# The beginning of an attention and MLP kernel, laid out anew: smaller loads, another order on every engine, more bank pairs, identity matmuls at the start

## Chip, core and metric

One core of a Trainium2 chip runs the program. The metric is the device time of one execution in microseconds (us), as the median of several. "Span" is the time from the first to the last instruction of one profiled execution.

## What is computed

Three stages, all float32. B = 8 batches, 8 heads, 576 tokens, head size 64; 4608 tokens of width 512.

```python
def sm_attn(qq, kk, vv): ...      # softmax(qq kk^T / 8) vv, per batch and head
p_packed = sm_attn(p, k, v)       # 32 packed queries
x = sm_attn(q, p_packed, p_packed)
xn = x / sqrt(mean(x * x) + 1e-6) * rms_g
g = xn @ w_gate                   # 512 x 1536
x = (g * sigmoid(g) * (xn @ w_val)) @ w_o       # 1536 x 512
out = (((x @ w1) * (x @ w2)) @ w3) @ w_out      # 1024 wide inside
```

## The kernel before, in words

Each float32 operand of a large product is split into two parts of a type that TensorE takes in one pass: `hi` is a cast by ScalarE (ACT), `lo` is the difference to the original, by VectorE (DVE). A product is then three matmuls: hi·hi, hi·lo, lo·hi.

**The main loop** (L639 to L648) goes over 8 batches, 2 halves of 288 tokens and 12 chunks of the inner width. A slot is `into` (12 matmuls: gate and value of a chunk, psum banks 0 and 1), then `outof` of the slot before (12 matmuls, banks 2 to 5) and at most one **item**, a small piece of the attention of this or the next batch. ACT and DVE make the activation between them. After the loop come the two 1024-wide products (`into2`, `outof2`).

**Items** run in a written order (`FIRST_ITEMS` and `SLOT_ITEM`), and all use the same pair of psum banks, 6 and 7. `xy_full` counts items that TensorE (PE) has finished, `xy_free` those that have been read out. S1 is the scores of the packed queries, AT their transposes, PV the product with v, PT another transpose, S2 the second scores, Z and SS the sums of squares, M (six for each batch) the product of the packed values with a piece of w_gate or w_val. M pieces are split into `m_hi` (ACT) and `m_lo` (DVE), which is what `into` multiplies with.

**The inverse rms** goes from engine to engine: SS on PE, `ssum` and `ms` on DVE (L831, L836), two small operations on GpSimd (POOL, L414 and L418) that give `rr`, a store of `rr` to memory and a load spread over 128 partitions as `r_sb` (`spread_r`, L278 and L282, both issued by SyncE, SP), the scaling of `a2T` on POOL (L425), then `a2_hi` on ACT (L696) and `a2_lo` on DVE (L894). `into` of the first slot waits for `a2_lo` (L534).

**The beginning** (L611 to L638) is what is changed. w3 · w_out is multiplied out once to a 1024 x 512 matrix, in two halves of 4 banks each; `fuse(half, c)` is one step of 12 matmuls of 512 columns, and there are 8 steps for each half. Between the steps stand the items of batch 0 and the first two of batch 1. `fuse_split` (ACT L701, L703; DVE L900, L903) makes hi and lo of chunk c of w_out (`wout`, half 0 only) and of w3 (`w3a`, `w3b`). `wf_evict` reads a finished half out of psum, `store_wf` writes it to memory. `wo_split` splits chunk f of w_o, which is loaded into the region of the fuse operands once `fuse_done` says that both halves are through (L323).

All DMAs are issued by SP in one written order (L301 to L330) and go through one queue. In the beginning that is: k and p of batch 0, w_out and w3 in loads of two chunks (512 KB), v, q, then k and p of batch 1, w3's second half, four pieces of w_gate and w_val (`w_in`, 1 MB each, four buffers), v and q of batch 1, the first store of the product, `spread_r(0)`, two more w_in pieces, and w_o in three loads of 1 MB.

## Time and profile before

| what | value |
|---|---|
| median of 3 runs | 1412.66 us (1412.58 to 1413.02) |
| the profiled execution, whole | 1412.07 us |
| its span | 1410.3 us |
| mean granted TensorE clock | 0.999 of full |
| TensorE busy | 1386.3 us, 98% of the span |
| DVE, ACT, POOL busy | 43%, 29%, 10% |
| moved by DMA | 129.13 MB, 92 GB/s on average |

The rows further down come from one profiled execution. Times are from the start of the span. A row of the timeline gives the start, the duration, engine, source line, operation, what it writes and reads, and in square brackets the idle time of that engine ahead of it and what ended this idle time. Matmuls are pipelined, so a listed duration is longer than the distance to the next start; the distance is what counts. Most float32 matmuls outside the split products appear as two instructions each.

### The profile page before, as it was taken

Reading aid. Unit: us, or ns where it says so; the run is one execution under the profiler, and the core shown is the slowest. Engines: PE = TensorE matmul, PEld = TensorE weight load, DVE = VectorE, ACT = ScalarE, POOL = GpSimd, SP = SyncE. Lnnn points to the kernel's source line nnn. Section 1 sums busy time; section 2 is a strip of 40 time slices with the busy share of each in tenths; the row PEclk is TensorE's granted clock in tenths of the full one; section 3 lists DMA queues with packets and bytes.
Section 4 is the critical chain, followed back from the end, with each engine's and each line's share of the span. In section 5 each row is a group of like instructions: output and inputs, shape, how many; then the busy total and the mean of one; then the engine's idle time right before and its main releaser. Section 6 shows DMA issues by size and latency. Waiting matters only on the chain.

```text
span 1410.3 us, 22634 instructions
## 1 busy us (share of the span) xinstructions
PE 1386.3 (98%) x9688; PEld 1194.8 (85%) x9688; DVE 605.7 (43%) x1095; ACT 406.9 (29%) x803; POOL 141.4 (10%) x137
## 2 busy tenths in 40 slices
PE   7989999999999999999999999999999999999999
PEld 5679899898898998988989988888888888888887
DVE  3657556565565565655655632212212111212111
ACT  4253342433423424334233422111111111111111
POOL 0100100001001000010012030220202020202000
PEclk9999999999999999999999999999999999999999
DMA  9882451533424515323024130101011010100000
GB/s 332 233 314 82 129 163 41 196 106 93 165 86 128 163 39 197 107 92 131 18 69 167 47 107 0 60 0 60 0 60 45 16 60 0 60 0 30 0 30 30
DMA packets 59155, 129.13 MB, mean 92 GB/s; under 512 B 3504, under 2 KB 12720, under 8 KB 57264
## 3 DMA queue, kind: packets, MB, share of 16 engines
q1 hardware_dynamic: 59056, 127.70, 27.6%
q8 instruction: 76, 1.25, 0.4%
q14 instruction: 23, 0.19, 0.0%
HBM read 106.69 MB, written 20.99 MB: 91 GB/s over the span
## 4 chain that ended last, share of the span: by engine, by line
PE 95%; DVE 3%; ACT 1%; issue 1%; DMA 0%; SPq 0%; DVEq 0%; ACTq 0%
PE psum L586 9%; PE psum L584 9%; PE psum L585 9%; PE psum L546 8%; PE psum L565 7%; PE psum L567 7%; PE psum L566 7%; PE psum L547 7%; PE psum L548 7%; PE psum L606 5%; PE psum L605 5%; PE psum L604 5%; PE psum L513 3%; PE psum L500 1%; PE psum L526 1%; PE psum L467 1%
## 5 line engine op out<-in xcount | busy, mean ns | idle before, releaser
L546 PE MATMUL psum<-a_hi,m_hi 128*128 128x288 f32 x768 | 240.7, 313 | 0.4
L565 PE MATMUL psum<-g_hh,wo_hi 128*128 128x288 f32 x768 | 227.4, 296 | 4.5 <-DVE g_res L921 2.6
L547 PE MATMUL psum<-a_lo,m_hi 128*128 128x288 f32 x768 | 226.7, 295 | 0.0
L548 PE MATMUL psum<-a_hi,m_lo 128*128 128x288 f32 x768 | 226.3, 295 | 0.0
L567 PE MATMUL psum<-g_hh,wo_lo 128*128 128x288 f32 x768 | 226.0, 294 | 0.0
L566 PE MATMUL psum<-g_hl,wo_hi 128*128 128x288 f32 x768 | 225.9, 294 | 0.0
L1012 DVE TENSOR_TENSOR b_h<-b_s,psum 128x512 f32<-128x512 f32 x72 | 49.5, 688 | 408.9 <-PE psum L586 408.9
L584 PE MATMUL psum<-xh,w_hi 128*128 128x512 f32 x576 | 224.1, 389 | 0.0
L585 PE MATMUL psum<-xl,w_hi 128*128 128x512 f32 x576 | 224.1, 389 | 0.0
L586 PE MATMUL psum<-xh,w_lo 128*128 128x512 f32 x576 | 224.1, 389 | 0.0
L546 PEld LDWEIGHTS psum<-a_hi,m_hi 128*128 128x128 f32 x768 | 144.4, 188 | 50.6 <-issue 46.6
L565 PEld LDWEIGHTS psum<-g_hh,wo_hi 128*128 128x128 f32 x768 | 144.1, 188 | 7.6 <-issue 6.1
L787 ACT CAST g_hh<-g_h 128x288 fp32r<-128x288 f32 x192 | 83.2, 433 | 223.2 <-DVE g_h L982 223.2
L547 PEld LDWEIGHTS psum<-a_lo,m_hi 128*128 128x128 f32 x768 | 144.9, 189 | 0.7
L548 PEld LDWEIGHTS psum<-a_hi,m_lo 128*128 128x128 f32 x768 | 144.7, 188 | 0.0
L567 PEld LDWEIGHTS psum<-g_hh,wo_lo 128*128 128x128 f32 x768 | 144.2, 188 | 0.0
L566 PEld LDWEIGHTS psum<-g_hl,wo_hi 128*128 128x128 f32 x768 | 144.1, 188 | 0.0
L976 DVE SCALAR_TENSOR_TENSOR g_s<-g_s,psum 128x288 f32<-128x288 f32 x192 | 86.4, 450 | 124.4 <-ACT g_s L783 122.7
L586 PEld LDWEIGHTS psum<-xh,w_lo 128*128 128x128 f32 x576 | 108.1, 188 | 22.4
L585 PEld LDWEIGHTS psum<-xl,w_hi 128*128 128x128 f32 x576 | 108.1, 188 | 22.4
L584 PEld LDWEIGHTS psum<-xh,w_hi 128*128 128x128 f32 x576 | 108.1, 188 | 22.3
L796 ACT COPY b_s<-psum 128x512 f32<-128x512 f32 x72 | 42.4, 589 | 275.2 <-PE psum L586 275.2
(109 smaller groups left out, 1737.2 us busy)
## 6 DMA issues: line engine op xcount, KB each, us to landing
w_in<-in_w_gate SPq DMA_DIRECT2D x24, 1024.0 KB, 5.3
w_in<-in_w_val SPq DMA_DIRECT2D x24, 1024.0 KB, 5.3
kT<-in_kT SPq DMA_DIRECT2D x8, 1152.0 KB, 7.7
v_sb<-in_v SPq DMA_DIRECT2D x8, 1152.0 KB, 7.2
qT<-in_qT SPq DMA_DIRECT2D x16, 576.0 KB, 3.8
y_scratch<-g_res SPq DMA_DIRECT2D x16, 576.0 KB, 3.2
x_raw<-y_scratch SPq DMA_DIRECT2D x9, 1024.0 KB, 7.6
out<-b_res SPq DMA_DIRECT2D x8, 1024.0 KB, 5.2
```

The source lines that it names most:

```text
L546: nc.tensor.matmul(in_ps[which], hi, a2_hi[:, t, par, :], start=par == 0, stop=False)
L547: nc.tensor.matmul(in_ps[which], hi, a2_lo[:, t, par, :], start=False, stop=False)
L548: last = nc.tensor.matmul(in_ps[which], lo, a2_hi[:, t, par, :], start=False, stop=par == 1)
L565: nc.tensor.matmul(out_ps[m], hi, hh[:], start=f == 0, stop=False)
L566: nc.tensor.matmul(out_ps[m], hi, hl[:], start=False, stop=False)
L567: last = nc.tensor.matmul(out_ps[m], lo, hh[:], start=False, stop=f == FC - 1)
L584: nc.tensor.matmul(dst, hi, xh[t % 2][:, kc, :], start=kc == 0, stop=False)
L585: nc.tensor.matmul(dst, hi, xl[t % 2][:, kc, :], start=False, stop=False)
L586: last = nc.tensor.matmul(dst, lo, xh[t % 2][:, kc, :], start=False, stop=kc == KC - 1)
L604: nc.tensor.matmul(out2_ps[m], hh[:, cols], wf_hi[:, f, :], start=f == 0, stop=False)
L787: nc.scalar.copy(g_hh[f % 2][:], g_h[:]).then_inc(hh_ready, 1)
L976: nc.vector.scalar_tensor_tensor(out=g_s[:], in0=g_s[:], scalar=1.0, in1=in_ps[0], op0=ALU.add, op1=ALU.mult).then_inc(u_ready, 1)
```

## The change

The arithmetic is the same. The beginning is ordered anew on all engines:

- w_out and w3 are loaded chunk by chunk (256 KB, a semaphore each); the first chunk goes ahead of k and p; three w_in pieces go ahead of batch 1's k, and the fifth (`load_w_in(0, 4)`) ahead of `spread_r(0)`. w_o is loaded in four pieces, the first of one chunk.
- `WARM` = 18 matmuls of the 128x128 identity with itself stand at PE's start, into bank 5.
- `fuse` can do a step in two halves of two banks; the items are spread between them. `fuse_done` is counted for each bank, so that banks are read out one by one.
- Two items of the beginning use banks 0 and 1 (S1 part 1, AT part 1), and two use banks 4 and 5 (M parts 0 and 2); `pair_users` gives what each item waits for.
- M part 0 goes ahead of SS; the last M part is followed by two fuse steps, where before it was followed by S1 of batch 1; S1 part 1 of batch 1 goes behind the first `into`.
- ACT and DVE do the casts of the next fuse chunk ahead of the copies of an item; `shift1` and `exp1` of batch 1 and the splits of w_o come about a slot later.

The diff, cut to its core (the semaphores of the smaller loads, and the bank arguments of the items' readers on ACT and DVE, are left out):

```diff
...
-       ("Z", 0, 0), ("Z", 0, 1), ("SS", 0, 0), ("M", 0, 0), ("M", 0, 1), ("M", 0, 2), ("M", 0, 3),
+       ("Z", 0, 0), ("Z", 0, 1), ("M", 0, 0), ("SS", 0, 0), ("M", 0, 1), ("M", 0, 2), ("M", 0, 3),
        ("S1", 1, 0), ("S1", 1, 1)]
+FIRST_BANK = {("S1", 0, 1): 0, ("AT", 0, 1): 0, ("M", 0, 0): 4, ("M", 0, 2): 4}
+WARM = 18
+WO_LOADS = [slice(0, 1), slice(1, 4), slice(4, 8), slice(8, 12)]
...
+def pair_users(number):
+    users, last = {}, {}
+    for item in sorted(number, key=number.get):
+        bank = FIRST_BANK.get(item, 6)
+        users[item] = last.get(bank, 0)
+        last[bank] = number[item] + 1
+    return users
...
-    def load_fuse(half, i):
-        rows = slice(2 * i, 2 * i + 2)
+    def load_fuse(half, c):
         if half == 0:
-            sp.dma_start(wout_raw[:, rows, :], wout_v[:, rows, :]).then_inc(wout_loaded[i], 16)
-        sp.dma_start(w3_raw[half][:, rows, :], w3_v[:, rows, BANK * half:BANK * (half + 1)]).then_inc(w3_loaded[half][i], 16)
+            sp.dma_start(wout_raw[:, c, :], wout_v[:, c, :]).then_inc(wout_loaded[c], 16)
+        sp.dma_start(w3_raw[half][:, c, :], w3_v[:, c, BANK * half:BANK * (half + 1)]).then_inc(w3_loaded[half][c], 16)
+    load_fuse(0, 0)
     load_kp(0)
-    load_fuse(0, 0)
-    load_fuse(0, 1)
+    for c in range(1, 4):
+        load_fuse(0, c)
     load_v(0)
-    load_fuse(0, 2)
-    load_fuse(0, 3)
+    load_fuse(0, 4)
     load_q(0, 0)
     sp.dma_start(gcol[:], g_d).then_inc(g_loaded, 16)
+    load_fuse(0, 5)
+    load_fuse(0, 6)
     load_q(0, 1)
+    load_fuse(0, 7)
+    for c in range(FC2):
+        load_fuse(1, c)
+    for part in range(3):
+        load_w_in(0, part)
     load_kp(1)
-    for i in range(4):
-        load_fuse(1, i)
-    for part in range(4):
-        load_w_in(0, part)
+    load_w_in(0, 3)
     load_v(1)
     load_q(1, 0)
     load_q(1, 1)
     store_wf(0)
+    load_w_in(0, 4)
     spread_r(0)
-    for part in range(4, PIECES):
-        load_w_in(0, part)
-    sp.wait_ge(fuse_done, 2)
-    for i in range(3):
-        rows = slice(4 * i, 4 * i + 4)
+    load_w_in(0, 5)
+    sp.wait_ge(fuse_done, 2 * 4)
+    for i, rows in enumerate(WO_LOADS):
         sp.dma_start(wo_raw[:, rows, :], wo_v[:, rows, :]).then_inc(wo_loaded[i], 16)
-        if i == 0:
+        if i == 1:
             store_wf(1)
...
         if kind == "M":
+            if bank == 4:
+                pe.wait_ge(wf_dve, 2)
             piece = PIECES * a + part
...
-    def fuse(half, c):
+    def fuse(half, c, rows=(0, 1, 2, 3)):
         pe.wait_ge(w3_lo_ready, FC2 * half + c + 1)
         if half == 0:
             pe.wait_ge(wout_lo_ready, c + 1)
-        for r in range(4 * half, 4 * half + 4):
+        for m in rows:
+            r = 4 * half + m
             if c == 0 and r >= 6:
-                pe.wait_ge(wf_act, 2)
-            cols = slice(P * (r - 4 * half), P * (r - 4 * half + 1))
+                pe.wait_ge(wf_act, r - 5)
+            cols = slice(P * m, P * (m + 1))
             hi, lo, dst = w3_hi[half][:, c, cols], w3_lo[half][:, c, cols], psum[:, fuse_bank[r], :]
...
             last = nc.tensor.matmul(dst, lo, wout_hi[:, c, :], start=False, stop=c == FC2 - 1)
-        if c == FC2 - 1:
-            last.then_inc(fuse_done, 1)
+            if c == FC2 - 1:
+                last.then_inc(fuse_done, 1)
     def into(b, t, f, n):
         if f == 0:
             pe.wait_ge(a2lo_ready, 2 * b + t + 1)
         if t == 0 and f % 4 == 0:
             freed(pe, "M", b, f // 4 * 2 + 1)
-        if n == 0:
-            pe.wait_ge(wf_act, 4)
         for which in range(2):
+            if n == 0:
+                pe.wait_ge(wf_act, 3 + which)
             if n:
                 pe.wait_ge((u_ready, h_ready)[which], n)
             cols = slice(P * (f % 4), P * (f % 4 + 1))
...
     pe.wait_ge(const_ready, 3)
+    for _ in range(WARM):
+        nc.tensor.matmul(psum[:, 5, 0:P], ident[:], ident[:], start=True, stop=True)
+    fuse(0, 0)
     item("S1", 0, 0)
     item("S1", 0, 1)
-    fuse(0, 0)
     fuse(0, 1)
+    fuse(0, 2)
     item("AT", 0, 0)
-    fuse(0, 2)
     item("AT", 0, 1)
-    fuse(0, 3)
+    fuse(0, 3, (0, 1))
     item("PV", 0, 0)
+    fuse(0, 3, (2, 3))
+    item("PT", 0, 0)
     fuse(0, 4)
-    item("PT", 0, 0)
+    item("S2", 0, 0)
     fuse(0, 5)
-    item("S2", 0, 0)
-    fuse(0, 6)
+    fuse(0, 6, (0, 1))
     item("S2", 0, 1)
+    fuse(0, 6, (2, 3))
     fuse(0, 7)
-    fuse(1, 0)
+    fuse(1, 0, (0, 1))
     item("Z", 0, 0)
+    fuse(1, 0, (2, 3))
     fuse(1, 1)
-    fuse(1, 2)
+    fuse(1, 2, (0, 1))
     item("Z", 0, 1)
-    fuse(1, 3)
+    item("M", 0, 0)
+    fuse(1, 2, (2, 3))
     item("SS", 0, 0)
-    for part in range(4):
-        fuse(1, 4 + part)
+    for part in range(1, 4):
+        fuse(1, 2 + part)
         item("M", 0, part)
+    fuse(1, 6)
+    fuse(1, 7)
     item("S1", 1, 0)
-    item("S1", 1, 1)
     for b in range(B):
         for t in range(2):
...
                 into(b, t, f, n)
                 if n:
                     outof(n - 1)
+                else:
+                    item("S1", 1, 1)
                 it = slot_item(b, t, f)
                 if it:
                     item(*it)
...
     def fuse_split(half, c):
         if half == 0:
-            act.wait_ge(wout_loaded[c // 2], 16)
+            act.wait_ge(wout_loaded[c], 16)
             nc.scalar.copy(wout_hi[:, c, :], wout_raw[:, c, :]).then_inc(wout_hi_ready, 1)
-        act.wait_ge(w3_loaded[half][c // 2], 16)
+        act.wait_ge(w3_loaded[half][c], 16)
         nc.scalar.copy(w3_hi[half][:, c, :], w3_raw[half][:, c, :]).then_inc(w3_hi_ready, 1)
     def wo_split(f):
-        act.wait_ge(fuse_done, 2)
-        act.wait_ge(wo_loaded[f // 4], 16)
+        act.wait_ge(wo_loaded[next(i for i, rows in enumerate(WO_LOADS) if f < rows.stop)], 16)
         nc.scalar.copy(wo_hi[:, f, :], wo_raw[:, f, :]).then_inc(wo_hi_ready, 1)
     def wf_evict(half):
-        act.wait_ge(fuse_done, half + 1)
         for r in range(2):
+            act.wait_ge(fuse_done, 4 * half + r + 1)
             nc.scalar.copy((wf_first, wf_second)[half][:, r, :], psum[:, fuse_bank[4 * half + r], :]).then_inc(wf_act, 1)
...
+    fuse_split(0, 0)
+    fuse_split(0, 1)
     item("S1", 0, 0)
     item("S1", 0, 1)
-    fuse_split(0, 0)
-    fuse_split(0, 1)
+    fuse_split(0, 2)
     exp1(0, 0)
     exp1(0, 1)
-    fuse_split(0, 2)
+    fuse_split(0, 3)
     item("AT", 0, 0)
-    fuse_split(0, 3)
     item("AT", 0, 1)
     fuse_split(0, 4)
     item("PV", 0, 0)
...
     fuse_split(1, 1)
     wf_evict(0)
     exp2(0, 1)
-    for c in range(2, FC2):
+    for c in range(2, 6):
         fuse_split(1, c)
     item("M", 0, 0)
+    fuse_split(1, 6)
+    fuse_split(1, 7)
     item("M", 0, 1)
     item("M", 0, 2)
+    item("M", 0, 3)
     a2_split(0, 0)
     wf_evict(1)
-    item("M", 0, 3)
+    item("S1", 1, 0)
     act.wait_ge(wf_stored[0], 16)
-    item("S1", 1, 0)
-    item("S1", 1, 1)
-    wo_split(0)
     for b in range(B):
         for t in range(2):
             for f in range(FC):
...
                 prev = before(b, t, f)
                 if prev and slot_item(*prev):
                     item(*slot_item(*prev))
-                if b + 1 < B and (t, f) in ((0, 1), (0, 2)):
-                    exp1(b + 1, f - 1)
+                if b + 1 < B and t == 0 and f - (2 if b == 0 else 1) in (0, 1):
+                    exp1(b + 1, f - (2 if b == 0 else 1))
...
                 if n:
                     act.wait_ge(h_ready, n)
-                if n + 1 < FC:
-                    wo_split(n + 1)
+                if n < FC:
+                    wo_split(n)
                 act.wait_ge(h_ready, n + 1)
+                if n == 0:
+                    item("S1", 1, 1)
...
     def wf_evict(half):
-        dve.wait_ge(fuse_done, half + 1)
         for r in range(2, 4):
+            dve.wait_ge(fuse_done, 4 * half + r + 1)
             nc.vector.tensor_copy((wf_first, wf_second)[half][:, r, :], psum[:, fuse_bank[4 * half + r], :]).then_inc(wf_dve, 1)
...
     fuse_split(0, 0)
+    fuse_split(0, 1)
     shift1(0)
-    fuse_split(0, 1)
+    fuse_split(0, 2)
     sums1(0)
-    for c in range(2, 7):
+    for c in range(3, 7):
         fuse_split(0, c)
     item("S2", 0, 0)
     shift2(0, 0)
...
     shift2(0, 1)
     fuse_split(1, 1)
     sums2(0, 1)
+    item("Z", 0, 0)
     normalize2(0, 1)
+    fuse_split(1, 2)
     wf_evict(0)
-    item("Z", 0, 0)
-    fuse_split(1, 2)
     fuse_split(1, 3)
     item("Z", 0, 1)
+    item("M", 0, 0)
     fuse_split(1, 4)
     item("SS", 0, 0)
-    for c in range(5, FC2):
-        fuse_split(1, c)
-    for part in range(3):
-        item("M", 0, part)
+    item("M", 0, 1)
+    fuse_split(1, 5)
+    fuse_split(1, 6)
+    item("M", 0, 2)
+    fuse_split(1, 7)
+    item("M", 0, 3)
     a2_split(0, 0)
     wf_evict(1)
-    item("M", 0, 3)
-    wo_split(0)
     for b in range(B):
         for t in range(2):
             for f in range(FC):
...
-                if b + 1 < B and (t, f) == (0, 0):
+                if 0 < b < B - 1 and (t, f) == (0, 0):
                     shift1(b + 1)
                 if b + 1 < B and (t, f) == (0, 3):
...
-                if n + 1 < FC:
-                    wo_split(n + 1)
+                if n < FC:
+                    wo_split(n)
                 dve.wait_ge(hh_ready, n + 1)
+                if n == 1:
+                    shift1(1)
                 if b + 1 < B and (t, f) in ((0, 9), (1, 0)):
                     sums2(b + 1, t)
                 if b + 1 < B and (t, f) == (1, 10):
```

## Rows read from the trace of the kernel before

**Rows 1.** The page's section 1: busy time, share and instructions of each engine.
```profile
PE 1386.3 (98%) x9688; PEld 1194.8 (85%) x9688; DVE 605.7 (43%) x1095; ACT 406.9 (29%) x803; POOL 141.4 (10%) x137
```

**Rows 2.** Windows: stretch, length, busy of PE, PEld, DVE, ACT, POOL; clock, DMA share, GB/s.
```profile
40.00:45.00 5.00, 4.70 (x21) 3.55 (x20) 4.83 (x8) 1.29 (x3) 0.00 (x0) 1.00 1.12 391
...
70.00:80.00 10.00, 6.72 (x67) 3.57 (x64) 4.36 (x5) 4.99 (x8) 2.30 (x2) 0.88 0.96 333
...
160.00:300.00 140.00, 139.35 (x1353) 123.56 (x1351) 79.95 (x156) 54.85 (x115) 6.79 (x8) 1.00 0.43 139
```

**Rows 3.** Timeline of PE, its start: first items, first fuse steps.
```profile
7.02 1.21 PE L467 MATMUL psum<-kT,pT 64*32 64x288 f32 x16 [7.02 <-DMA kT<-in_kT]
...
12.88 0.79 PE L526 MATMUL psum<-wout_hi,w3a_hi 128*128 128x512 f32 x1 [2.65 <-DVE w3a_lo L903]
...
16.03 0.47 PE L527 MATMUL psum<-wout_lo,w3a_hi 128*128 128x512 f32 x1
```

**Rows 4.** Timeline of PE, the stalls in the middle of the beginning.
```profile
39.18 0.50 PE L526 MATMUL psum<-wout_hi,w3a_hi 128*128 128x512 f32 x1 [0.22 <-DVE w3a_lo L903]
...
42.53 0.50 PE L526 MATMUL psum<-wout_hi,w3b_hi 128*128 128x512 f32 x1 [0.30 <-DVE w3b_lo L903]
...
50.86 0.50 PE L526 MATMUL psum<-wout_hi,w3b_hi 128*128 128x512 f32 x1 [1.57 <-DVE w3b_lo L903]
```

**Rows 5.** Timeline of PE, end of the beginning, first slots of the loop.
```profile
76.44 0.72 PE L467 MATMUL psum<-kT,pT 64*32 64x288 f32 x16 [2.43 <-DVE m_lo L840]
78.01 1.21 PE L467 MATMUL psum<-kT,pT 64*32 64x288 f32 x16 [0.85 <-ACT sc L661]
...
84.88 0.40 PE L565 MATMUL psum<-g_hh,wo_hi 128*128 128x288 f32 x1 [1.08 <-DVE g_hl L995]
```

**Rows 6.** Timeline of PE: four 128-column float32 instructions, and the next start.
```profile
34.84 0.49 PE L495 MATMUL psum<-ppT 64*128 64x128 f32 x4
35.26 0.50 PE L526 MATMUL psum<-wout_hi,w3a_hi 128*128 128x512 f32 x1
```

**Rows 7.** Timelines of ACT and DVE from first cast to `shift1`.
```profile
10.88 0.62 ACT L701 CAST wout_hi<-wout_raw 128x512 fp32r<-128x512 f32 x1
...
12.74 1.35 DVE L846 TENSOR_REDUCE nmax<-sc 128x2 f32<-128x1152 f32 x1
```

**Rows 8.** DMA issues in short windows: output, input, count, size, us from issue to landing.
```profile
w3a_raw<-in_w3T SPq DMA_DIRECT2D x1, 512.0 KB, 16.6
...
qT<-in_qT SPq DMA_DIRECT2D x1, 576.0 KB, 18.2
...
wf_scratch<-wf_first SPq DMA_DIRECT2D x1, 1024.0 KB, 10.1
...
r_scratch<-rr SPq DMA_DIRECT2D x1, 2.2 KB, 1.4
...
r_sb<-r_scratch SPq DMA_DIRECT2D x1, 288.0 KB, 5.2
```

**Rows 9.** Timeline of SP's queue: issue times of the transfers of rows 8.
```profile
6.75 0.48 SPq L299 DMA_DIRECT2D w3a_raw<-in_w3T  x1
...
37.77 1.62 SPq L264 DMA_DIRECT2D qT<-in_qT  x2
49.64 0.38 SPq L293 DMA_DIRECT2D wf_scratch<-wf_first  x1
62.78 0.33 SPq L278 DMA_DIRECT2D r_scratch<-rr  x1
```

**Rows 10.** Timelines of POOL, ACT and DVE: the end of the rms chain.
```profile
69.46 2.84 POOL L425 TENSOR_TENSOR a2T<-a2T,r_sb 128x576 f32<-128x576 f32 x2 [6.71 <-DMA r_sb<-r_scratch]
...
71.04 0.68 ACT L696 CAST a_hi<-a2T 128x576 fp32r<-128x576 f32 x1
...
72.32 0.75 DVE L894 TENSOR_TENSOR a_lo<-a2T,a_hi 128x576 fp32r<-128x576 f32 x1
```

**Rows 11.** The tile r_sb over the whole trace: its landings.
```profile
DMA to landing us min/median/max: 3.2/3.4/5.2
```

More of the change, by code:

```diff
@@ L181, in build @@
         out_ps = [psum[:, 2 + m, 0:HALF] for m in range(4)]
-        xy = [psum[:, 6, :], psum[:, 7, :]]
         in2_ps = [[psum[:, n, :] for n in pair] for pair in ((0, 1), (6, 7))]
@@ L191, in build @@
         w_in_loaded = [sem(f"w_in_loaded{i}") for i in range(W_BUFS)]
-        wout_loaded = [sem(f"wout_loaded{i}") for i in range(4)]
-        w3_loaded = [[sem(f"w3_loaded{h}{i}") for i in range(4)] for h in range(2)]
+        wout_loaded = [sem(f"wout_loaded{i}") for i in range(FC2)]
+        w3_loaded = [[sem(f"w3_loaded{h}{i}") for i in range(FC2)] for h in range(2)]
         wout_hi_ready, wout_lo_ready = sem("wout_hi_ready"), sem("wout_lo_ready")
         w3_hi_ready, w3_lo_ready = sem("w3_hi_ready"), sem("w3_lo_ready")
-        wo_loaded = [sem(f"wo_loaded{i}") for i in range(3)]
+        wo_loaded = [sem(f"wo_loaded{i}") for i in range(len(WO_LOADS))]
         fuse_done, wf_act, wf_dve, wf_stored = sem("fuse_done"), sem("wf_act"), sem("wf_dve"), [sem(f"wf_stored{i}") for i in range(2)]
@@ L221, in build, with banks @@
         number = item_numbers()
+        users = pair_users(number)
+        def banks(kind, a, part):
+            return FIRST_BANK.get((kind, a, part), 6)
         def full(eng, kind, a, part):
@@ L457, in item @@
             def item(kind, a, part):
-                n = number[kind, a, part]
+                n, bank = users[kind, a, part], banks(kind, a, part)
                 if n:
                     pe.wait_ge(xy_free, n)
+                xy = [psum[:, bank, :], psum[:, bank + 1, :]]
                 if kind == "S1":
@@ L658, in item @@
             def item(kind, a, part):
+                bank = banks(kind, a, part)
                 if kind == "S1":
                     full(act, "S1", a, part)
-                    nc.scalar.copy(sc[:, :, HALF * part:HALF * (part + 1)], psum[:, 6:8, 0:HALF]).then_inc(xy_free, 1)
+                    nc.scalar.copy(sc[:, :, HALF * part:HALF * (part + 1)], psum[:, bank:bank + 2, 0:HALF]).then_inc(xy_free, 1)
                 if kind == "AT":
                     full(act, "AT", a, part)
-                    nc.scalar.copy(a1T[:, part, :].rearrange("p (a n) -> p a n", a=2), psum[0:TP, 6:8, 0:3 * P]).then_inc(xy_free, 1)
+                    nc.scalar.copy(a1T[:, part, :].rearrange("p (a n) -> p a n", a=2), psum[0:TP, bank:bank + 2, 0:3 * P]).then_inc(xy_free, 1)
                 if kind == "PV":
@@ L667, in item @@
                     act.wait_ge(rden1_ready, a + 1)
-                    nc.scalar.activation(pp[:, 0:DH], xy[0][:, 0:DH], ACT.Copy, scale=rden1[:, 0:1])
-                    nc.scalar.activation(pp[:, DH:2 * DH], xy[1][:, 0:DH], ACT.Copy, scale=rden1[:, 1:2]).then_inc(xy_free, 1)
+                    nc.scalar.activation(pp[:, 0:DH], psum[:, bank, 0:DH], ACT.Copy, scale=rden1[:, 0:1])
+                    nc.scalar.activation(pp[:, DH:2 * DH], psum[:, bank + 1, 0:DH], ACT.Copy, scale=rden1[:, 1:2]).then_inc(xy_free, 1)
                 if kind == "PT":
                     full(act, "PT", a, part)
-                    nc.scalar.copy(ppT[:], xy[0][:, 0:P]).then_inc(xy_free, 1)
+                    nc.scalar.copy(ppT[:], psum[:, bank, 0:P]).then_inc(xy_free, 1)
                 if kind == "M":
@@ L678, in item @@
                         act.wait_ge(wf_stored[1], 16)
-                    nc.scalar.copy(m_hi[group][:, which, :, :], psum[:, 6:8, :]).then_inc(m_hi_ready, 1)
+                    nc.scalar.copy(m_hi[group][:, which, :, :], psum[:, bank:bank + 2, :]).then_inc(m_hi_ready, 1)
             def exp1(a, par):
@@ L810, in item @@
             def item(kind, a, part):
+                bank = banks(kind, a, part)
                 if kind == "S2":
@@ L839, in item @@
                     group, which = divmod(part, 2)
-                    nc.vector.tensor_tensor(m_lo[group][:, which, :, :], psum[:, 6:8, :], m_hi[group][:, which, :, :].bitcast(F32),
+                    nc.vector.tensor_tensor(m_lo[group][:, which, :, :], psum[:, bank:bank + 2, :], m_hi[group][:, which, :, :].bitcast(F32),
                                             ALU.subtract).then_inc(xy_free, 1)
```

## The prediction

> **What bounds the kernel now.** I read the page's busy times first: TensorE is busy 1386.3 of 1410.3 us [rows 1], so only some 24 us can be won without taking matmuls away. Then the windows: from 160 to 300 us PE is busy 139.35 of 140, while 70 to 80 us has only 6.72 of 10, and DMA moves 391 GB/s at 40 to 45 us, a share above 1 [rows 2]. So the idle time lies in the beginning, and there the DMA queue is full as well. The timeline of PE shows where it goes. PE waits 7.02 us for k, and after S1 another 2.65 for the first split operand [rows 3]; 0.22, 0.30 and 1.57 us for `w3_lo` [rows 4]; 2.43 us for `m_lo` of the last M part, 0.85 for a copy, 1.08 for `g_hl` [rows 5]. Last come the timelines of SP, POOL, ACT and DVE with the landing times, for what could be late next.
>
> I measure everything at one mark: the start of the first `outof`, 84.88 us [rows 5]. Behind it PE is full, so what the mark moves, the end moves.
>
> **The work on PE.** From the first fuse matmul (12.88) to the mark are 72.0 us. In them are stalls of 0.22 + 0.30 + 1.57 + 2.43 + 0.85 + 1.08 = 6.45 us. Half clock (1.2 GHz) costs more: the eight matmuls from 12.88 to 16.3 start 0.43 us apart, where 0.23 is normal: 1.5 us; the second S1 of batch 1 takes 1.2 for 0.65, and the seven matmuls behind it 0.24 for 0.13: 1.3 us with a little of the first S1 [rows 3, 5]. That leaves 72.0 - 6.45 - 1.5 - 1.3 = 62.75 us of full-speed work. The change puts the two S1 of batch 0 inside this stretch, where the first fuse step now stands ahead of them: 2 x 0.65 = 1.3, in all 64.05 us. No fuse matmul is taken away; a step in two halves costs nothing more that a row shows, and one item more between steps costs about 0.1 us (the first matmul behind an item starts 0.34 instead of 0.23 us apart), inside my rounding.
>
> **When the first fuse step starts.** Before, k and p (1.24 MB) had landed at 7.02 [rows 3]. Now the first pair of chunks (0.52 MB) is ahead of them; 0.72 MB less at 391 GB/s is 1.85 us [rows 2], so it lands at 5.2. From first cast to first fuse matmul it took 12.88 - 10.88 = 2.0 us [rows 3, 7]: 7.2 us. Meanwhile 18 identity matmuls run, two instructions each. Four such instructions take 0.42 us at full clock [rows 6], so one matmul is 0.21, and 0.42 at half. Before, the clock rose after PE had been working from 12.88 to about 16.1 [rows 3]; if it rises as long after 1.6 us (the constants are done at 1.5), that is 7 or 8 at half and 10 or 11 at full clock, done at about 7.1. They cost nothing, and save the 1.5 us of half clock. If the clock doesn't rise they end at 1.6 + 18 x 0.42 = 9.2: 2 us, with the half clock some 3.5.
>
> **The next steps.** S1 now has two bank pairs, so the second doesn't wait for the copy of the first. `shift1` (1.35 us [rows 7]) can only start when both copies are through, and now stands ahead of the split of chunk 2: fuse step 0 ends at 9.95 and S1 at 11.3, the copies at 12.0, `shift1` at 13.4, `lo` of chunk 2 at 14.7; PE has finished step 1 at 14.1. A new stall of about 0.6 us, and behind it on DVE stands only the next split. The middle stalls (2.1 us) go: DVE's work between S2 and Z is the same, and PE has half a step to a step (1.4 to 2.7 us) more ahead of each Z; if that cover isn't enough, they come back, 2.1 us. The 2.43 and 0.85 go: two fuse steps (5.5 us) now cover the last M split. The 1.08 goes: `shift1` of batch 1 no longer stands ahead of `g_hl`.
>
> If PE's own work were last everywhere, the mark would stand at 7.2 + 64.05 + 0.6 = 71.85. So **PE alone gives 84.88 - 71.85 = 13.0 us**.
>
> **What is late next: the rms chain, through the DMA queue.** `into` of slot 0 can't start before `a2_lo`, which comes through `rr`, a store, a spread load, POOL, ACT and DVE. Before, `rr` was done and its store issued at 62.78, when the queue was empty; the store took 1.4 us [rows 8, 9]. Now SS comes some 9 us sooner (start 5.7, stalls 2.1, clock 1.5, one fuse step less and an M more ahead of it, and so on), so `rr` is ready at about 54. But loads land in the order of issue, and they don't depend on PE's speed: SP had the last of batch 1's q issued at about 39 (the second of the two issues at 37.77), and it landed 18.2 us later, at 57.2; the store of the product behind it, issued at 49.64, took 10.1 and landed at 59.7 [rows 8, 9]. The change moves the same bytes ahead of that point. Then it puts one more ahead of `spread_r(0)`: SP issues `load_w_in(0, 4)` when M part 0 is done, at about 46, so its 1.05 MB follow at 391 GB/s: 2.7 us, to 62.4. The store of `rr`, issued at 54, lands behind them, at about 62.7. Then the spread load takes 5.2 as before (it has again a w_in behind it at once), or 3.4 as in the other batches [rows 11]: 67.9. From that landing to the end of `a_lo` is 69.46 to 71.04, then 0.68 and 0.75, 3.0 us [rows 10]: `a2_lo` at **70.9**.
>
> PE is at this place at 71.85 less `into` twice (2 x 12 x 0.133 = 3.2) less S1 (0.65), 68.0. It waits 2.9 us. In before, 2.43 and 0.85 us of idle time were followed by the fall to 1.2 GHz and 1.3 us lost [rows 5]; I take 1.6 here (3.2 us at half), as the wait is in one piece. Mark: 70.9 + 3.85 + 1.6 = 76.35. **Gain 84.88 - 76.35 = 8.5 us.**
>
> What else is moved: banks 0 and 1 are read out by ACT behind `a2_hi`, 2 x 0.53 us, one before each half of `into`; that fits beside DVE's `a_lo`. The second store of the product is issued when DVE has read its banks, about 72.2, and lands near 77; M part 4 needs it at 79. w_o's first chunk is issued when fuse ends (about 67) and lands by 72 behind `r_sb` and a w_in. Nothing there is late, with 2 us to spare; if it is, the cost is under 1 us. Behind SP's waits for `rr` and the store stand only w_in 5, w_o and the second store, so these shift with them.
>
> A rule that speaks against the change: the Trainium skill, "DMA: Bandwidth & Descriptors", section Bandwidth, wants DMAs of 1 MiB for 75% of peak, with about 2.0 us fixed for each; by it a 256 KB load would take 2.6 us, and the 24 small loads would hold 48 us of fixed time, if none of it overlapped. A gap of that kind is priced from rows below and is the third rival.
>
> The rows bound that gap: between k (7.02) and the last `w3a` load (issued 6.75, landed 16.6 later, at 23.35) nine loads with 5.37 MB landed [rows 3, 8, 9]. At 391 GB/s these take 13.7 of the 16.3 us, so a load leaves 0 to 0.29 us. The change adds 12 loads: 0 to 3.5 us on the queue's tail. I take 0, since the loads of k, v and w3 keep the DMA share at 1 while they run, and v with its own shape can hold the whole 2.6 us.
>
> **Rivals.**
> 1. *PE last everywhere* (the queue drains sooner than I think, or the spread load takes 3.2 and the clock holds). For it: it takes only 2.9 us of idle. Gain 13.0: 1399.7. Against: the landing at 59.7 is a row and needs nothing of PE.
> 2. *The chain later still*: the 12 further loads at the upper bound, 3.5 us, give 1407.7 at most.
> 3. *Slower: the small loads leave large gaps.* A 2.2 KB transfer alone takes 1.4 us [rows 8]. If each of the 12 further loads left 1.4 us uncovered, the queue's tail, and with it `a2_lo`, would move by 16.8 us: 1404.2 + 16.8 = 1421.0. It decides for slower from (8.5 + 2.8) / 12 = 0.94 us for each load. Against it: the 0.29 above.
> 4. *The identity matmuls don't do what they are for*: 3.5 us on PE's way, which then stands at 75.35, still ahead of the chain's 76.35: 1404 again.
>
> **How the numbers follow.** The profiled execution's whole time is 1412.07, its span 1410.3, and the median 1412.66, 0.6 above. Span after: 1401.8; execution 1403.6; by the median 1404.2. I predict 1404.0. Forecast (with rival 4, which lies inside it; 1401.5 to 1406) 0.58; rival 1 0.25; rival 2 0.11; rival 3 0.03; 0.03 for a result within 0.2% by a mixture of stalls. The range 1399.0 to 1408.0 takes in rivals 1 and 2. A measurement of this kernel tells 0.2%, 2.8 us, from no change: faster 0.94, same 0.03, slower 0.03.
>
> **What would show it.** In PE's timeline of after: identity matmuls from 1.6 us, spacing halved before they end; first fuse matmul near 7.2; a stall near 14 us of 0.6 on `w3a_lo`; none over 0.3 up to 65; then one of 2 to 3 us ahead of L546's successor that `a_lo` ends, at about 71, with matmuls at half clock behind it; the mark at 76. In SP's and the DMA rows: `rr` ready near 54 and its store landing some 8 us later. Wrong if that store lands within 2 us, if PE waits for chunks between fuse steps, or if stalls appear behind the mark.

## The result, and the profile after

| | before | after |
|---|---|---|
| median of 6 executions each | 1412.78 us | 1405.81 us (1400.3 to 1408.23) |
| ratio, 95% interval | | 0.9946 (0.9929 to 0.9964), 7.6 us less |
| profiled execution, span | 1412.07, 1410.3 us | 1408.23, 1406.4 us |
| mark: start of the first `outof` | 84.88 us | 81.07 us |
| mark to the end of the span | 1325.4 us | 1325.3 us |

The changed kernel is faster: 7.0 us by the medians and 7.6 by the ratio, where the forecast was 8.7 from the median. Its executions differ by 8 us where those of before differ by 1, and the profiled one is the slowest of them. What lies behind the mark didn't change between these two profiles. So the effect is in where the mark stands; whether the spread is too, the next run of the same kernel tells.

The timeline of PE of the changed kernel (columns as in the rows ahead of the prediction): its start, which answers to [rows 3], and the end of the beginning, which answers to [rows 5].

```profile
1.57 5.97 PE L640 MATMUL psum<-ident 128*128 128x128 f32 x36 [1.57 <-POOL ones L412]
7.30 0.47 PE L554 MATMUL psum<-wout_hi,w3a_hi 128*128 128x512 f32 x1
...
12.92 0.50 PE L554 MATMUL psum<-wout_hi,w3a_hi 128*128 128x512 f32 x1 [1.49 <-DVE w3a_lo L943]
...
67.95 0.71 PE L489 MATMUL psum<-kT,pT 64*32 64x288 f32 x16
74.36 0.61 PE L574 MATMUL psum<-a_hi,m_hi 128*128 128x288 f32 x1 [5.70 <-DVE a_lo L934]
74.77 0.45 PE L575 MATMUL psum<-a_lo,m_hi 128*128 128x288 f32 x1
...
81.07 0.29 PE L593 MATMUL psum<-g_hh,wo_hi 128*128 128x288 f32 x1
```

The first fuse step starts at 7.3 instead of 12.9 us. Of the stalls of [rows 4] none is left. Then PE waits 5.7 us for `a_lo` (`a2_lo` in the prediction), ahead of the first `into`, where the kernel before had waited for `m_lo` and a copy shortly ahead of it. The matmuls behind it start 0.24 us apart, where 0.13 is the distance at full clock. The windows of the changed kernel show the same, against 70 to 80 us in [rows 2]; the clock is the column ahead of the DMA share, 0.67 from 70 to 80 us.

```profile
60.00:70.00 10.00, 8.67 (x62) 5.54 (x60) 2.56 (x3) 1.02 (x1) 0.00 (x0) 1.00 0.54 148
70.00:80.00 10.00, 5.64 (x33) 4.45 (x34) 4.32 (x7) 4.17 (x8) 2.75 (x2) 0.67 0.81 278
80.00:90.00 10.00, 10.00 (x91) 8.00 (x90) 7.70 (x13) 6.61 (x13) 0.00 (x0) 0.99 1.04 377
```

Why `a_lo` is late is told by SP's queue and the landing times of the changed kernel, which answer to [rows 8] and [rows 9].

```profile
48.45 0.38 SPq L292 DMA_DIRECT2D w_in<-in_w_gate  x1
54.11 2.52 SPq L297 DMA_DIRECT2D r_scratch<-rr  x1
65.76 0.34 SPq L301 DMA_DIRECT2D r_sb<-r_scratch  x1
```

```profile
qT<-in_qT SPq DMA_DIRECT2D x1, 576.0 KB, 21.5
...
wf_scratch<-wf_first SPq DMA_DIRECT2D x1, 1024.0 KB, 18.0
...
w_in<-in_w_gate SPq DMA_DIRECT2D x1, 1024.0 KB, 17.1
...
r_scratch<-rr SPq DMA_DIRECT2D x1, 2.2 KB, 11.6
...
r_sb<-r_scratch SPq DMA_DIRECT2D x1, 288.0 KB, 5.1
```

`rr` is ready at 54.1, 8.7 us sooner than before. Its 2.2 KB take 11.6 us where they took 1.4 [rows 8]. The w_in piece issued ahead of them at 48.45 landed 17.1 us later, at 65.55, and they landed at 65.7. The last q landed at 39.0 + 21.5 = 60.5 (57.2 before), the first store of the product at 45.0 + 18.0 = 63.0 (59.7 before).

### The profile page after: what moved, and what is told of

Its sections match the earlier page's. It is cut to its first block, busy times and chain, and to the rows that moved or that the text cites. A ratio compares the mean times of both kernels' runs of the same rounds, so it can differ in the third digit from the quotient of the medians.

```text
span 1406.4 us, 22711 instructions
## 1 busy us (share of the span) xinstructions
PE 1390.1 (99%) x9724; PEld 1200.5 (85%) x9724; DVE 606.2 (43%) x1095; ACT 407.4 (29%) x803; POOL 139.4 (10%) x137
## 3 DMA queue, kind: packets, MB, share of 16 engines
q8 instruction: 77, 1.26, 0.4%
## 4 chain that ended last, share of the span: by engine, by line
PE 94%; issue 2%; DVE 2%; ACT 1%; DMA 1%; SPq 0%; POOL 0%; DVEq 0%; POOLq 0%
PE psum L613 9%; PE psum L612 9%; PE psum L614 9%; PE psum L574 8%; PE psum L593 7%; PE psum L575 7%; PE psum L576 7%; PE psum L595 7%; PE psum L594 7%; PE psum L633 5%; PE psum L634 5%; PE psum L632 5%; PE psum L538 3%; PE psum L522 1%; PE psum L501 1%
```

## The experiments

Each was timed against the kernel before on its own chip, whose median lay between 1412.3 and 1412.8 us throughout. `a_again`, `e1_swap`, `e2_actq` and `e3_fill` shared one chip, `e5_512` to `e11` one, `e12` to `e14` one, and `e15_best_warm0` had its own. Single executions of one kernel spread by up to 8 us, so a median of four or five can mislead; where two kernels are compared below, their intervals against before are given if they overlap. The expectations speak of a *queue theory*: on one queue a transfer lands only when those issued ahead of it have landed.

| kernel | median | single executions | mark, profiled |
|---|---|---|---|
| `a_again` (changed kernel) | 1405.69 | 1400.58 to 1406.27 | 79.09 |
| `e1_swap` | 1403.03 | 1400.39 to 1404.17 | 76.99 |
| `e2_actq` | 1402.30 | 1400.45 to 1404.57 | 75.17 |
| `e3_fill` | 1404.29 | 1404.04 to 1406.44 | 77.33 |
| `e5_512` | 1400.28 | 1399.48 to 1402.65 | 75.53 |
| `e9_defer` | 1401.84 | 1400.93 to 1404.20 | 74.62 |
| `e10_defer_warm0` | 1401.59 | 1399.82 to 1402.40 | 73.77 |
| `e11_defer_onepair` | 1404.90 | 1404.44 to 1405.63 | 77.79 |
| `e12_512_defer` | 1400.13 | 1399.93 to 1400.63 | 71.89 |
| `e14_512_swap` | 1399.93 | 1399.49 to 1400.62 | 72.05 |
| `e13_before_256` (on before) | 1412.31 | 1412.07 to 1413.10 | 85.40 |
| `e15_best_warm0` | 1401.30 | 1401.03 to 1403.02 | 73.76 |

### The changed kernel once more

> The changed kernel itself, once more, so that the others have it on their own chip. Single executions lay between 1400.3 and 1408.2 us. If the wait for a_lo and the clock make this spread, the profiled execution has the wait at 5 to 6 us (68.6 to 74.3 before) and either one or two stretches of some 3.4 us at 1.2 GHz behind it; if the start or a later part of the kernel makes it, the wait and the mark (start of the first outof, 81.1) stand still while the end moves.

In its profiled execution PE finished S1 of batch 1 at 67.6 us, a microsecond sooner than in the first profile, waited 5.4 us and had the mark at 79.09:

```profile
73.00 0.61 PE L574 MATMUL psum<-a_hi,m_hi 128*128 128x288 f32 x1 [5.40 <-DVE a_lo L934]
...
79.09 0.30 PE L593 MATMUL psum<-g_hh,wo_hi 128*128 128x288 f32 x1
```

Span less mark is 1325.4 again. So between the two profiles, 2.0 us apart at the mark, a later part of the kernel is ruled out as the source of the difference: 1.4 us are the start of the first `into`, 0.6 the clock behind it (6.1 us from there to the mark, 6.7 in the first profile). Two of the eleven executions of this kernel are at 1400.3 and 1400.6. No profile shows such an execution. By their times the mark stood at 72 to 73.4 (with 1325.4 to 1326.4 behind it, as in the profiles below), about where PE's own work alone puts it. By that estimate `a_lo` was there 4 to 6 us sooner, as it was in `e3_fill` below.

### One transfer less ahead of `rr`

```diff
+            spread_r(0)
             load_w_in(0, 4)
-            spread_r(0)
             load_w_in(0, 5)
```

> The fifth w_in piece is issued behind the spread of rr instead of ahead of it. Queue theory: the store of rr then lands behind the first store of the product alone, at about 63 instead of 65.7, so a_lo is ready 2.7 us sooner (71.6), PE waits about 3 instead of 5.7 us; median 2.7 us below the changed kernel, up to 4.5 if less of the work behind it runs at half clock. Rival, the wait is set by something else of the chain (POOL, DVE's place): no change, within 0.5 us.

2.7 us faster than `a_again` by the medians, as the queue theory gave, but the times alone don't prove it: the intervals against before overlap (0.9916 to 0.9941, and 0.9927 to 0.9954). The timeline of SP and of PE:

```profile
53.92 0.33 SPq L297 DMA_DIRECT2D r_scratch<-rr  x1
62.85 0.32 SPq L301 DMA_DIRECT2D r_sb<-r_scratch  x1
...
71.38 0.40 PE L574 MATMUL psum<-a_hi,m_hi 128*128 128x288 f32 x1 [2.90 <-DVE a_lo L934]
```

The store of `rr` landed at 62.8 instead of 65.7, and PE waited 2.9 us instead of 5.7. What shows the piece's own share is the distance to the first store of the product. In four profiles with the w_in piece between the two (`after`, `a_again`, `e3_fill`, `e5_512`) the store of `rr` landed 2.7 to 2.8 us behind that store; in the two with the piece behind (`e1_swap`, `e14_512_swap`) 0.2 us. So the piece is worth 2.5 us, and it is one part of the delay only.

### Another queue

```diff
             item("M", 0, 1)
+            act.wait_ge(rr_ready, 1)
+            act.dma_start(r_dram[:, 0:S].rearrange("o (p j) -> (o p) j", j=NT), rr[:]).then_inc(r_stored, 16)
             item("M", 0, 2)
+            act.wait_ge(r_stored, 16)
+            act.dma_start(r_sb[:], r_dram[:, 0:S].to_broadcast([P, S])).then_inc(r_loaded, 16)
```

(and `spread_r(0)` taken out of SP's order)

> The store of rr and the spread load are issued by ACT, between M parts 1, 2 and 3, so they don't stand in SP's queue. Queue theory (the order in one queue is what holds the store back): it lands within 3 us of its issue, the spread load in 4 to 8 us beside the other traffic, a_lo before 68.6, so PE doesn't wait: the mark falls from 81.1 to about 72.5, span 1406.4 - 8.6 = 1397.8, median about 1398 to 1399. Rival, the DMA engines are simply full until 65.5 whichever queue asks: the store still lands at 63 to 66 and the time stays within 1 us of the changed kernel.

Both forecasts were too simple. The timeline of ACT's queue, and the landing times of the two:

```profile
53.32 0.39 ACTq L793 DMA_DIRECT2D r_scratch<-rr  x1
59.60 0.35 ACTq L796 DMA_DIRECT2D r_sb<-r_scratch  x1
```

The store landed after 6.3 us, not 11.6 and not 1.4, and the spread load took 6.5 instead of about 5. The second queue got round the order of the first, but not round its traffic. Part of that traffic is the edit's own doing: SP no longer waited for `rr` and issued the sixth w_in piece at 53.3 instead of 66.1, beside the store and ahead of the spread load. The median fell by 3.4 us of the 8.6 that the queue theory allowed (intervals 0.9914 to 0.9941, for `a_again` 0.9927 to 0.9954).

### The clock alone

```diff
             item("S1", 1, 0)
+            for _ in range(24):
+                nc.tensor.matmul(psum[:, 5, 0:P], ident[:], ident[:], start=True, stop=True)
```

> 24 matmuls of the identity with itself (0.215 us each at full clock, 5.2 us) are put into PE's wait for a_lo, into a bank that is free; nothing else changes. Clock theory: the wait itself stays (a_lo at 74.3), but the clock stays at 2.4 GHz, so into, S1 and into behind it take 4.1 instead of 6.7 us; median 2.5 to 3 us below the changed kernel, and the spread of single executions shrinks. Rival, the half clock costs nothing because g_hl and the load of w_o would be late anyway: within 0.5 us.

PE's timeline:

```profile
67.85 5.62 PE L675 MATMUL psum<-ident 128*128 128x128 f32 x48
73.23 0.38 PE L574 MATMUL psum<-a_hi,m_hi 128*128 128x288 f32 x1
...
77.33 0.30 PE L593 MATMUL psum<-g_hh,wo_hi 128*128 128x288 f32 x1
```

The granted clock stayed at full speed, and the mark followed the end of the filling by 4.1 us (73.23 to 77.33), where in the two profiles of the changed kernel `into`, S1 and `into` took 6.7 and 6.1 (74.36 to 81.07, 73.00 to 79.09). So the half clock behind the wait costs 2.0 to 2.6 us in an execution that has the wait.

The kernel's time gained nothing that can be told from noise: 1.4 us by the medians, but the intervals are 0.9932 to 0.9956 and, for `a_again`, 0.9927 to 0.9954. The expectation's "the wait itself stays" failed as well: `a_lo` was ready at 68.8 in this execution, and the filling held PE until 73.2. It takes from the good executions what it gives to the bad ones. Four of five executions lie within 0.5 us, but a filling that hides when `a_lo` comes would do that too, so this run doesn't show that the clock makes the spread.

### Loads of 512 KB again

```diff
             def load_fuse(half, c):
+                if c % 2:
+                    return
+                rows = slice(c, c + 2)
                 ...
-                sp.dma_start(w3_raw[half][:, c, :], w3_v[:, c, BANK * half:BANK * (half + 1)]).then_inc(w3_loaded[half][c], 16)
+                sp.dma_start(w3_raw[half][:, rows, :], w3_v[:, rows, BANK * half:BANK * (half + 1)]).then_inc(w3_loaded[half][c // 2], 16)
```

> The changed kernel with w_out and w3 loaded two chunks at a time (512 KB) as before, 12 loads fewer, everything else kept. Queue theory with a gap for each load: the last q load landed at 60.5 us, 3.3 us later than in the kernel before; if the 12 further loads are the cause, it lands at about 57.2 again, a_lo comes about 3 us sooner and the median falls 2 to 4 us below the changed kernel's 1405.7, unless the first fuse steps wait longer for their pairs (up to 1.5 us on PE, which the wait for a_lo hides). Rival, the later tail comes from the new order or from the execution: q still lands near 60, median within 1 us.

5.4 us faster than the changed kernel by the medians, 3.7 us by the ratios of `e5_512` and `a_again` (intervals against before: 0.9902 to 0.9929, for the changed kernel 0.9929 to 0.9964 and 0.9927 to 0.9954: they no more than touch). The last q landed at 36.9 + 19.9 = 56.8 instead of 60.5, the store of `rr` at 61.8 instead of 65.7. In the windows, 0 to 20 us, first the changed kernel, then this one; the last number is GB/s:

```profile
0.00:20.00 20.00, 16.85 (x114) 13.93 (x115) 7.60 (x17) 8.86 (x16) 0.83 (x9) 1.00 0.89 244
```

```profile
0.00:20.00 20.00, 17.73 (x119) 14.81 (x120) 7.44 (x17) 9.50 (x17) 0.83 (x9) 1.00 0.90 290
```

In these two profiles 46 GB/s less is 0.9 MB, 2.4 us at 391 GB/s: most of the 3.9 us by which the store of `rr` came later could have been lost there. But the rate of this window doesn't explain the landings alone. `a_again` moved 269 GB/s in it and `e3_fill` 268, and their stores of `rr` landed at 64.8 and 61.6.

The end of the queue can be compared in nine profiles, since the first store of the product stands behind the same loads in all of them. It landed at 63.0, 62.6, 62.1, 61.2 and 58.9 us with small loads in the new order (`after`, `e1_swap`, `a_again`, `e2_actq`, `e3_fill`), and at 59.0 and 57.9 with 512 KB (`e5_512`, `e14_512_swap`). In the old order it was 59.7 and 58.7 (`before`, `e13_before_256`). So small loads in the new order mostly cost 2 to 5 us there, and in one execution of five nothing.

### Small loads in the old order

```diff
             def load_fuse(half, i):
-                rows = slice(2 * i, 2 * i + 2)
+                for c in (2 * i, 2 * i + 1):
                 ...
```

(the kernel before, w_out and w3 loaded chunk by chunk)

> The kernel before with w_out and w3 loaded chunk by chunk (12 loads more, 256 KB each) in the same order, nothing else changed. Queue theory: the last q load lands about 3.3 to 4 us later (60.5 to 61 instead of 57.2), but rr is only ready at 62.8, so a_lo moves by no more than 1 us and the time stays within 0.5 us of before; the first fuse step may start up to 1.3 us sooner on its smaller pair. Rival, the small loads are not what costs: q lands at 57 to 58.

The time is that of before, ratio 1.0 (0.9991 to 1.0009). But the queue theory's reason for it failed: q landed 16.8 us after its issue at about 39.2, at 56, no later than with 512 KB. Its window, which answers to the two above:

```profile
0.00:20.00 20.00, 10.01 (x55) 6.52 (x56) 6.06 (x15) 7.29 (x13) 0.83 (x9) 1.00 0.90 289
```

So twelve loads more don't cost 3.5 us by themselves; a cost shows in the new order only. What it is of that order that makes the difference (the pair ahead of k and p, or the mixing of small loads with v and q) no run separates. The same window of the profiles puts the rates in numbers: the eight with small loads in the new order moved 244 to 276 GB/s, the four with 512 KB in the new order 290 to 305, the two in the old order 284 and 289. Why it needs both, and why the amount differs from execution to execution, is open.

### The spread of `rr` ahead of v and q

```diff
             load_w_in(0, 3)
-            load_v(1)
-            load_q(1, 0)
-            load_q(1, 1)
             store_wf(0)
-            load_w_in(0, 4)
             spread_r(0)
+            load_w_in(0, 4)
             load_w_in(0, 5)
+            load_v(1)
```

(q of batch 1 behind the first two w_in pieces of batch 1)

> The spread of rr goes ahead of w_in 4, of v and q of batch 1, which aren't needed before 80 us: 4.6 MB less stand in the queue ahead of it. Queue theory: the store of rr is issued at 53.5 and lands within 2 us, as in the kernel before; a_lo is ready at about 64, no wait ahead of into; the mark stands at PE's own 72 to 72.5 and the median at 1399.5 to 1400, with a spread of single executions under 1 us. Rival, something else holds a_lo or the clock falls anyway: 1402 or more.

The store of `rr` took 1.4 us and `a_lo` was done at 64.6, with no wait of PE ahead of `into`, as forecast. The mark didn't follow. PE's timeline, and ACT's:

```profile
67.15 0.71 PE L489 MATMUL psum<-kT,pT 64*32 64x288 f32 x16
67.80 0.40 PE L574 MATMUL psum<-a_hi,m_hi 128*128 128x288 f32 x1
...
74.62 0.40 PE L593 MATMUL psum<-g_hh,wo_hi 128*128 128x288 f32 x1 [2.54 <-DVE g_hl L1037]
```

```profile
72.86 0.62 ACT L745 CAST wo_hi<-wo_raw 128x512 fp32r<-128x512 f32 x1 [3.50 <-DMA wo_raw<-in_w_o]
```

Now v of batch 1 stood ahead of w_o's first chunk. v landed at 72.4 (56.1 + 16.3) and the chunk at 72.85, and the chunk held the split of `g_hh` behind it on ACT. The full queue hadn't become shorter, another transfer had become the last. Against `a_again` the median is 3.9 us lower, but the intervals overlap (0.9912 to 0.9939, and 0.9927 to 0.9954).

### Banks, on this footing

```diff
-FIRST_BANK = {("S1", 0, 1): 0, ("AT", 0, 1): 0, ("M", 0, 0): 4, ("M", 0, 2): 4}
+FIRST_BANK = {}
```

> e9_defer with every item in banks 6 and 7 again. Theory: the second S1 waits for the copy of the first, 0.7 us, the second AT 0.8, and M part 0 and SS wait for DVE to read out Z and M, up to 2 us each, so 2 to 5 us slower than e9_defer. Rival, the order alone makes room enough: within 0.5 us of it.

3.1 us slower than `e9_defer`, and no single execution of one lies among those of the other. PE's timeline shows the waits one by one, each for a read-out of banks 6 and 7:

```profile
12.38 0.72 PE L489 MATMUL psum<-kT,pT 64*32 64x288 f32 x16 [0.88 <-ACT sc L699]
...
21.24 0.86 PE L494 MATMUL psum<-ident,sc 128*96 128x128 f32 x6 [0.89 <-ACT a1T L702]
...
49.43 1.09 PE L538 MATMUL psum<-w_in,ppTg 64*32 64x512 f32 x16 [0.85 <-DVE wz L866]
...
52.96 0.91 PE L526 MATMUL psum<-ident,wsum 128*96 128x128 f32 x6 [0.83 <-DVE m_lo L880]
```

They sum to 3.45 us, and PE reached S1 of batch 1 at 71.2 instead of 67.15. The mark came 3.2 us later. The bank pairs are worth 3 to 4 us of PE's own time.

### The identity matmuls

```diff
-WARM = 18
+WARM = 0
```

First on `e9_defer`, then on `e12_512_defer` (next section).

> e9_defer without the 18 identity matmuls. In the changed kernel the first operands were ready at 5.5 us and the matmuls held PE until 7.3; the next chunk only came at 12.2. Theory: step 0 then starts at 5.5 at half clock, and PE waits for chunk 1 or for shift1 as before, so the time is that of e9_defer within 0.5 us. Rival, the warm clock is worth what was forecast when PE is last everywhere: 1.5 to 3.5 us slower than e9_defer.

> e12_512_defer without the 18 identity matmuls. In e12 nothing waits behind S1 of batch 1, so PE's own path sets the mark, unlike in e9 and e10, where w_o's chunk did. In e10 PE stood at that S1 0.9 us sooner than in e9, since step 0 started at 5.6 instead of 7.5. If that holds: 0.5 to 1 us faster than e12, about 1399.2 to 1399.6. Rival, as forecast: the matmuls save 1.5 us of half clock and more, and without them it is slower, 1401.5 to 1403.5.

On `e9_defer` the time stayed, as forecast, and PE stood at S1 of batch 1 0.9 us sooner without them (66.22 for 67.15): the first operands were ready at 5.59, and the 18 matmuls hold PE until 7.0 to 8.4 (in ten profiles). The mark came 0.85 us sooner too, but in that execution PE ran at half clock behind its wait for `g_hl` (granted clock 0.83 from 70 to 80 us, 1.00 in `e9_defer`), and span less mark was 1326.8. On `e12_512_defer` the expectation was wrong: 1401.30 for 1400.13, 1.2 us slower. The intervals overlap (0.9912 to 0.9939, and 0.9899 to 0.9926) and the chips differ, but no single execution of one lies among those of the other, and PE's way shows it: S1 of batch 1 at 68.11 for 67.12. PE's timeline of the two kernels without them, `e10_defer_warm0` first:

```profile
5.59 0.77 PE L554 MATMUL psum<-wout_hi,w3a_hi 128*128 128x512 f32 x1 [5.59 <-DVE w3a_lo L943]
...
7.01 0.63 PE L554 MATMUL psum<-wout_hi,w3a_hi 128*128 128x512 f32 x1
```

```profile
7.33 0.77 PE L557 MATMUL psum<-wout_hi,w3a_hi 128*128 128x512 f32 x1 [7.33 <-DVE w3a_lo L946]
...
10.03 0.63 PE L557 MATMUL psum<-wout_hi,w3a_hi 128*128 128x512 f32 x1
```

The first pair of loads is twice as large in `e12`, so its operands come at 7.33 and not at 5.59. Step 0 took 4.5 us without the matmuls and 2.9 behind them (`e15`, `e12`), so they do save the 1.5 us of half clock. With small loads they cost more than that, since they hold PE 1.9 us past its operands (5.59 to 7.50); with large ones they fill a wait that is mostly there anyway, and hold PE 0.5 us past it (7.33 to 7.85).

### Both together

```diff
+            (load_fuse as in e5_512)
             load_w_in(0, 3)
             store_wf(0)
             spread_r(0)
             load_w_in(0, 4)
             load_w_in(0, 5)
             ...                          # w_o and the second store
+            load_v(1)
+            load_q(1, 0)
+            load_q(1, 1)
```

(`e12_512_defer`; `e14_512_swap` is `e5_512` with the two lines of `e1_swap` changed places)

> Loads of two chunks (512 KB) as in e5_512, and v and q of batch 1 behind the loads of w_o. In e9_defer v stood ahead of w_o's first chunk, which then landed at 72.85 and held g_hl and the first outof by 2.54 us. Queue theory: a_lo at about 62 to 64, w_o's chunk at 70, so neither waits: mark 72.0 to 72.6, median 1399.2 to 1399.8, spread of single executions under 1.5 us. Rival, there is a next wait just behind (M part 4, v or q too late for batch 1): median above 1400.5.

> e5_512 with the fifth w_in piece behind the spread of rr. a_lo comes 2.7 us sooner than in e5_512 (69.9 to 67.2), where PE's own work stands: median 1399.5 to 1400, the same as e12 within 0.5. Rival, e5_512 already hides it in most executions: no gain over its 1400.3.

Both reach 1400, 12.2 and 12.4 us under their own before, ratios 0.9912 (0.9899 to 0.9926) and 0.9911 (0.9897 to 0.9924), and single executions lie within 1.1 us. Both beat the changed kernel, by intervals that don't overlap. Neither can be told from `e5_512` (1400.28, 0.9902 to 0.9929): the large loads alone bring nearly all of it, and what moving the transfers adds is at most a smaller spread (0.7 and 1.1 us, for 3.2). `e14` came in where it was forecast, but its rival (no gain over `e5_512`) can't be ruled out; `e12` ended 0.3 us above its range, though its mark came at 71.89, forecast 72.0 to 72.6. PE's timeline of `e12`, then that of `e14_512_swap` with ACT's, which shows the next wait:

```profile
71.89 0.29 PE L596 MATMUL psum<-g_hh,wo_hi 128*128 128x288 f32 x1
...
79.04 1.09 PE L541 MATMUL psum<-w_in,ppTg 64*32 64x512 f32 x16 [1.01 <-DVE m_lo L883]
```

```profile
79.17 1.09 PE L541 MATMUL psum<-w_in,ppTg 64*32 64x512 f32 x16 [0.97 <-DVE m_lo L883]
```

```profile
76.84 1.02 ACT L720 CAST m_hi<-psum 128x1024 fp32r<-128x1024 f32 x1 [1.59 <-DMA wf_scratch<-wf_second]
```

The mark is at 72, but M part 4 has to wait on ACT until the second store of the product has left the region it is written to, and M part 5 behind it costs 1.0 us. Span less mark is 1326.4 in both, not 1325.4, so of the microseconds won at the mark one is lost again.

## Why the prediction was right

It was right in its sign, its range and its mechanism, and 1.8 us too low. The time that it named fits the median only: single executions lie from 1400.3 to 1408.2, and that spread it didn't foresee. The single steps, from PE's rows of the changed kernel:

- **PE's own work.** First fuse step at 7.2 us, measured 7.30; PE at `into` of slot 0 at 68.0, measured 68.6 and, in `a_again`, 67.6. The middle stalls, the 2.43, the 0.85 and the 1.08 went. Only the bank pairs and the identity matmuls were taken back by themselves; what the other moves on PE, ACT and DVE are worth is read from the stalls that are gone, and no run shows it. The value 7.2 was right for a wrong reason: the first operands were ready at 5.46, since their loads landed at 4.1 and not at 5.2, and what PE worked on until 7.3 was the identity matmuls, forecast to end at 7.1. Of the estimate that they "cost nothing, and save the 1.5 us" the second half held, and the first failed with small loads, by `e10`: they held PE 1.9 us past its operands.
- **A new stall of 0.6 us on step 2.** In `a_again` 0.70, on the operand forecast. In the first profile it was 1.49, one step sooner, because chunk 1 landed at 11.5, and nothing of it on step 2; another 0.48 stood at 23.7. That is one of the forecast's own signs of being wrong ("if PE waits for chunks between fuse steps"). It cost nothing, since it is inside the 5.7 us that PE waits later anyway.
- **The rms chain is late next.** Right, and this is what carried the forecast: `a_lo`, the place, the half clock behind it. `rr` was issued at 54.1, forecast 54.
- **The size of the wait.** The mark came at 81.07, 4.7 us later than 76.35. The term that was too small is "I take 0" for what the 12 further loads leave on the queue's tail, where its own bound was 0 to 3.5: q, the first store and the store of `rr` each landed 3.0 to 3.3 us late in the first profile (65.7 for 62.7). For the store of `rr` it was 2.1 in `a_again`, and in `e3_fill`, with the same loads, it was 1.1 us early (61.6). The rows of before couldn't show it, and `e13` shows that it isn't a price for each load: rival 2 had the right size, with only part of the cause. That the median lies between the forecast and rival 2 is an average over executions with and without this delay, and in part luck. Another 0.5 us is the end of the chain, where DVE's `a_lo` took 1.24 us for 0.75 (below), and 1.3 us the clock: two `into` and S1 at half speed nearly throughout, 6.7 us, where I took 5.45. In the median execution the mark stood near 78.5, by an estimate (1405.7 - 1.8 - 1325.4).
- **Rival 1**, PE last everywhere at 1399.7: two executions in eleven have about this time (no trace of them), and `e12` and `e14` make it the rule, at 1400.1 and 1399.9.
- **Rival 3**, slower: no sign of it. The rule of the Trainium skill ("DMA: Bandwidth & Descriptors", section Bandwidth) on small transfers points the right way for this order (`e5_512`). Its size is far off: the first store of the product landed 0 to 5 us later with small loads in the new order. The fixed 2.0 us for each DMA, which the same page of the Trainium skill gives in its section "Anatomy of one DMA — SWDGE (gpsimd) path" from DMAs issued by GpSimd, would make 24 us for the 12 further loads, by an estimate in which nothing overlaps. In the old order (`e13`) nothing of it shows.
- **Rival 4**, the clock doesn't rise under the identity matmuls: it didn't come about. Step 0 ran at full clock behind them in all ten profiles that have them, and it began at 7.0 to 8.4, where the rival had 9.2. Leaving them out altogether makes PE's way to S1 of batch 1 0.9 us shorter (`e10`) or 1.0 longer (`e15`).
- **M part 4 with 2 us to spare**: right at a mark of 76, and gone at 72, as `e14` shows.

## What to carry to other kernels

When a start-up is rewritten to keep one engine busy, write down when each small transfer of a dependent chain is issued and what stands in its queue ahead of it: here 2.2 KB waited 11.6 us behind megabytes that weren't needed for another 20 us. Moving one megabyte behind it brought it 2.5 us forward, and with v and q behind it as well, it took 1.4 us; but then the next transfer in the same queue was the last. The size of the loads mattered at least as much as their order: going back to 512 KB was the only single edit whose interval no more than touches that of the changed kernel.

The half clock behind a wait belongs to its price: a wait of 5.7 us cost 8.3. Filling the wait with other matmuls keeps the clock, but holds the engine back in the executions in which the wait is short. And a kernel whose time starts to vary, here from a spread of 1 us to one of 8, may have a transfer that decides the time in some executions and not in others.
